# Masking one head of the next unit ahead of VectorE's copies in the third and fifth step of a pair

## The chip, the cores and the metric

The kernel runs on 1 core of one Trainium2 chip. The metric is the device time of one execution in microseconds (us).

## What is computed

Attention over 4 x 8 heads (sequence 576, head dimension 64) with a threshold, then two mixing blocks. Only the attention matters here:

```python
scores = scale * np.matmul(q, k.transpose(0, 1, 3, 2))
thresh = np.max(scores, axis=-1, keepdims=True) - tau
scores = np.where(scores >= thresh, scores, -1000000000.0)
scores = scores - np.max(scores, axis=-1, keepdims=True)
attn = np.exp(scores)
attn = attn / (np.sum(attn, axis=-1, keepdims=True) + 1e-09)
return np.matmul(attn, v).astype(np.float32)
```

Its result goes through a token and a channel mixing block with ReLU, and through a gated convolution block (`x @ w_in`, three taps, sigmoid, `@ w_out`), all in float32.

## The kernel before, in words

Each engine has a program of its own, written out by hand; semaphores are the only link between them. The 32 heads are worked on as 16 **pairs** (k = 0 to 15, `PAIRS` = 16). A pair has 576 rows of queries, cut into five **units** t = 0 to 4: four full ones of 128 rows with two heads each, and a tail (t = 4) in which the 64 last rows of both heads share the 128 partitions, so that it counts as one head. A pair is one call of `body`, with five steps s = 0 to 4. `at.unit(n)` names the unit n steps into the pair; n = 5 and up are those of the next pair. Pairs 0 to 3 and 14 on are written out, 4 to 13 run in a loop, two at a time (an even and an odd one).

The stages of a unit, engine by engine:

- TensorE, `scores` (L1034, tail L1039): the scores of a unit into two pairs of banks of the tensor `score`, one pair per head. Each matmul waits on `max_done`, that is until VectorE has copied the same head of the unit before out of that bank.
- VectorE, `copy_out` (L876): one instruction per head takes the scores out of PSUM, scales and negates them into `negs`, and leaves the row's extreme in `neg_max`. It waits on `s_done` (the scores are there) and on `mask_done` (the buffer of two units ago is free).
- ScalarE, `exp_unit` (L624, L627): one exponential per head as soon as its copy is done, and behind the last the threshold `thresh` of the unit (one instruction for both heads), which signals `thr_done`.
- VectorE, `mask` (L893): one instruction per head compares `negs` with `thresh`, multiplies with the exponential, writes `prob` and adds up the row. It waits on `thr_done`, on `exp_done` for its head, and on `tail_turned` or `t_done`, by which TensorE says that it has turned the `prob` of two units ago.
- TensorE, `turn_probs` (L1060, tail L1069 to L1077): transposes `prob` head by head, each head when its mask is done (`mask_done`), into `turn_x` and `turn_y`. `turn_tails` (L1114) turns the columns of the tail.
- ScalarE, `drain_turned_probs` (L641): copies them to `probT`. Then TensorE multiplies with V in the next pair (`times_v`, L1129), and the result is turned, normalised (VectorE `normalise` L916, ScalarE `normalise_short` L695) and turned back.

In step s of a pair TensorE makes the scores of unit s + 2 and then turns unit s; VectorE copies unit s + 2 out and then masks unit s + 1; ScalarE drains unit s and then does the exponentials of unit s + 2. Behind this, the token mixing of two pairs is spread over the pairs: from k = 3 on in the odd ones its first product (`mix_hidden`, L1181), from k = 4 on in the even ones the second (`mix_out`, L1210). GpSimd splits the weights and the attention's results into high and low parts meanwhile (L440, L454, L477, L491, L498) and adds (L506).

VectorE's body sets the order of the work around the change:

```python
if two:
    copy_out(two)
if s == 4 and at.units:
    invert_sums(at)
if one:
    mask(one)
```

Of the kernel before, what the change touches and what calls it, by code (L numbers as in the profile page):

```python
# [25 lines left out]
def build(nc, qk_in, v_in, tau, w_tok1, w_tok2, w_ch1, w_ch2, w_in, conv_w, w_out, out):  # L26
# [11 lines left out]
    FULL = S // P  # L38
    TAIL = S - FULL * P
    NT = FULL + 1  # L40
# [154 lines left out]
    with ctx:  # L195
# [12 lines left out]
        def sem(name):  # L208
            return ctx.enter_context(nc.semaphore(name))
# [17 lines left out]
        thr_done = sem("thr_done")  # L227
        exp_done = sem("exp_done")
        mask_done = sem("mask_done")
        t_done = sem("t_done")  # L230
        tail_turned = sem("tail_turned")
# [6 lines left out]
        sum_done = sem("sum_done")  # L238
# [75 lines left out]
        def tiles_to(g, t):  # L314

            return TILES * g + min(2 * t, TILES)

        def slot_of(k, t):

            return (NT * k + t) % 2  # L320
# [536 lines left out]
        def _(dve):  # L857
# [9 lines left out]
            def copy_out(unit):  # L867

                g, k, t = unit
                i = slot_of(k, t)  # L870
                if NT * k + t >= 2:
                    before = (g, t - 1) if t >= 1 else (g - 1, FULL)
                    dve.wait_ge(mask_done, tiles_to(*before))
                dve.wait_ge(s_done, NT * g + t + 1)
                for h in range(2 if t < FULL else 1):
                    nc.vector.tensor_scalar(negs[:, i, h, :].rearrange("p (c s) -> p c s", c=2), raw_of[h], neg_scale[:, 0:1], None, ALU.mult, ALU.min,  # L876
                                            accum_out=neg_max[:, i, h:h + 1]).then_inc(max_done, 1)

            def mask(unit):

                g, k, t = unit
                i = slot_of(k, t)
                if NT * k + t >= 2:
                    if t == 1:
                        dve.wait_ge(t_done, NT * g)
                    else:
                        dve.wait_ge(tail_turned, FULL * g + max(t - 1, 0))
                if t == 0 and k >= 1:
                    dve.wait_ge(sum_done, g)
                dve.wait_ge(thr_done, NT * g + t + 1)  # L890
                for h in range(2 if t < FULL else 1):
                    dve.wait_ge(exp_done, tiles_to(g, t) + h + 1)
                    nc.vector.scalar_tensor_tensor(out=prob[:, i, h * S:(h + 1) * S], in0=negs[:, i, h, :],  # L893
                                                   scalar=thresh[:, i, h:h + 1], in1=exps[i][:, h, :],
                                                   op0=ALU.is_le, op1=ALU.mult,
                                                   accum_out=rowsum[:, 2 * t + h:2 * t + h + 1]).then_inc(mask_done, 1)

            def add_to_sums(at):

                dve.wait_ge(mask_done, TILES * (at.g + 1))  # L900
                nc.vector.tensor_scalar(rowsum_pos[:, :], rowsum[:, :], 1e-9, None, ALU.add).then_inc(sum_done, 1)

            def invert_sums(at):

                dve.wait_ge(sum_done, at.g + 1)
                nc.vector.reciprocal(rinv[at.par][:, :], rowsum_pos[:, :]).then_inc(inv_done, 1)

            def normalise(pair, k):

                dve.wait_ge(xa_done, pair + 1)  # L910
                dve.wait_ge(inv_done, pair + 1)
                if k >= 1:
                    dve.wait_ge(x_split, pair)
                    dve.wait_ge(xt_done, pair)
                halves = 2 * FULL
                nc.vector.tensor_tensor(x32[:, 0:FULL, :].rearrange("p t (h c) -> p (t h) c", h=2),  # L916
                                        out_t[:, :].rearrange("p (n c) -> p n c", c=D),
                                        rinv[k % 2][:, 0:halves].unsqueeze(2).broadcast_to([P, halves, D]), ALU.mult) \
                    .then_inc(x_done, 1)

            def split_first_u():
                dve.wait_ge(pv_done, PAIRS)
                for i in range(2):
                    k = slice(i * KM // 2, (i + 1) * KM // 2)
                    dve.wait_ge(u_hi_first, i + 1)
                    nc.vector.tensor_tensor(ul[0][:, k, :], uy[:, 0, k, 0:CHUNK], uh[0][:, k, :].bitcast(F32), ALU.subtract) \
                        .then_inc(u_lo_first, 1)

            first, second = (0, 0, 0), (0, 0, 1)
            copy_out(first)  # L930
            copy_out(second)
            mask(first)

            def body(at):
                for s in range(NT):
                    two, one = at.unit(s + 2), at.unit(s + 1)
                    if two:
                        copy_out(two)
                    if s == 4 and at.units:
                        invert_sums(at)  # L940
                    if one:
                        mask(one)
                    if s == 1 and at.k == PAIRS:
                        split_first_u()
                    if s == 3 and at.pv:
                        normalise(at.g - 1, at.k - 1)
                    if s == 3 and at.units:
                        add_to_sums(at)

            bodies(dve, body)  # L950


# [455 lines left out]
```

## Time and profile before

| | |
|---|---|
| median of 3 runs | 846.94 us (846.65 to 847.15) |
| the profiled execution | 847.35 us |
| its span, first to last instruction | 845.5 us |
| mean granted TensorE clock | 0.996 |
| TensorE matmuls busy | 823.7 us, 97% |
| VectorE busy | 417.7 us, 49% |
| ScalarE busy | 413.3 us, 49% |
| GpSimd busy | 257.5 us, 30% |
| L893, the masks | 144 times, 129.1 us, mean 929 ns |
| L876, the copies | 144 times, 112.7 us, mean 816 ns |
| L624, the exponentials | 144 times, 104.7 us |

Times in the profile count from the span's start. The pairs take the first 330 us or so, the channel mixing and the convolution block the rest. The granted clock is given as a share of 2.4 GHz: 1.00 is 2.4 GHz, 0.50 is 1.2 GHz. In a timeline a row is an instruction (or a run of equal ones, x2, x8): its start, its duration, and in brackets how long the engine was idle before it and what ended that. Durations include the time in the pipeline, so the next instruction of an engine can start a little before the end of the one before.

### The profile page before, as it was taken

Reading aid. Unit: us, or ns where it says so; the run is one execution under the profiler, and the core shown is the slowest. Engines: PE = TensorE matmul, PEld = TensorE weight load, DVE = VectorE, ACT = ScalarE, POOL = GpSimd, SP = SyncE. Lnnn points to the kernel's source line nnn. Section 1 sums busy time; section 2 is a strip of 40 time slices with the busy share of each in tenths; the row PEclk is TensorE's granted clock in tenths of the full one; section 3 lists DMA queues with packets and bytes.
Section 4 is the critical chain, followed back from the end, with each engine's and each line's share of the span. In section 5 each row is a group of like instructions: output and inputs, shape, how many; then the busy total and the mean of one; then the engine's idle time right before and its main releaser. Section 6 shows DMA issues by size and latency. Waiting matters only on the chain.

```text
span 845.5 us, 15190 instructions
## 1 busy us (share of the span) xinstructions
PE 823.7 (97%) x5656; PEld 670.9 (79%) x5656; DVE 417.7 (49%) x829; ACT 413.3 (49%) x914; POOL 257.5 (30%) x202
## 2 busy tenths in 40 slices
PE   8989999999999998899999999999999999999998
PEld 4657777777777767788888888888899999898996
DVE  6887878878878774401211211211214819155380
ACT  5877888878878884211211211211114727265461
POOL 0251223223323224460200200110391726428170
PEclk9999999999999999999999999999999999999999
DMA  9311111111111204000000000000320010100101
GB/s 267 110 47 48 49 48 47 47 47 47 47 47 49 61 2 150 1 1 0 1 1 1 0 1 1 1 0 1 137 63 2 1 51 1 50 13 0 50 0 62
DMA packets 20906, 32.70 MB, mean 39 GB/s; under 512 B 4416, under 2 KB 11136, under 8 KB 20864
## 3 DMA queue, kind: packets, MB, share of 16 engines
q1 hardware_dynamic: 20864, 32.13, 11.8%
q8 instruction: 28, 0.46, 0.2%
q14 instruction: 14, 0.11, 0.0%
HBM read 27.41 MB, written 4.72 MB: 38 GB/s over the span
## 4 chain that ended last, share of the span: by engine, by line
PE 92%; DVE 3%; ACT 2%; issue 2%; DMA 1%; POOL 0%; ACTq 0%; SPq 0%; DVEq 0%; POOLq 0%
PE score L1238 17%; PE score L1353 12%; PE score L1034 7%; PE out_t L1253 4%; PE turn_y L1253 4%; PE mixed L1253 4%; PE turn_x L1253 4%; PE out_t L1129 4%; PE out_t L1338 4%; PE mixed L1129 4%; PE mixed L1181 3%; PE turn_x L1060 3%; PE turn_y L1338 3%; PE mixed L1338 3%; PE turn_x L1338 3%
## 5 line engine op out<-in xcount | busy, mean ns | idle before, releaser
L956 DVE SCALAR_TENSOR_TENSOR h<-score,h 128x512 fp32r<-128x512 f32 (+1 forms) x60 | 38.3, 638 | 243.5 <-ACT h L726 243.5
L726 ACT ACTIVATE h<-score 128x512 fp32r<-128x512 f32 (+1 forms) x60 | 33.3, 555 | 250.5 <-PE score L1238 250.5
L876 DVE TENSOR_SCALAR_CACHE_REDUCE negs<-score,neg_scale 128x576 f32<-128x576 f32 x144 | 112.7, 816 | 60.1 <-PE score L1034 44.8
L893 DVE SCALAR_TENSOR_TENSOR prob<-negs,thresh,exps 128x576 f32<-128x576 f32 x144 | 129.1, 929 | 0.3 <-ACT thresh L627 0.3
L624 ACT ACTIVATE exps<-negs,neg_max 128x576 f32<-128x576 f32 x144 | 104.7, 772 | 1.9 <-DVE negs L876 1.2
L1034 PE MATMUL score<-qk 64*128 64x288 f32 x512 | 85.6, 435 | 2.6 <-DVE negs L876 2.1
L1238 PE MATMUL score<-uh,w1l 128*128 128x512 f32 (+1 forms) x240 | 86.8, 368 | 0.0
L1238 PE MATMUL score<-uh,w1h 128*128 128x512 f32 (+1 forms) x240 | 86.8, 368 | 0.0
L1238 PE MATMUL score<-ul,w1h 128*128 128x512 f32 (+1 forms) x240 | 86.8, 368 | 0.0
L592 POOL TENSOR_TENSOR zl<-z,zh 128x512 fp32r<-128x512 f32 x32 | 54.2, 1693 | 98.7 <-ACT zh_t L814 98.7
L1034 PEld LDWEIGHTS score<-qk 64*128 64x128 f32 x512 | 47.4, 189 | 28.8 <-issue 13.7
L514 POOL TENSOR_TENSOR ul<-uy,uh 128x256 fp32r<-128x256 f32 (+6 forms) x7 | 16.7, 2398 | 161.7 <-ACT uh L713 161.7
L996 DVE SCALAR_TENSOR_TENSOR conv<-hpad,cw,conv 128x576 f32<-128x576 f32 x32 | 27.2, 849 | 77.4 <-ACT conv L827 77.3
L1060 PEld LDWEIGHTS turn_x<-ident,prob 64*128 64x128 f32 x512 | 41.1, 139 | 20.1 <-issue 14.6
L641 ACT ACTIVATE probT<-turn_x 128x512 f32<-128x512 f32 x64 | 38.1, 596 | 35.4 <-PE turn_y L1060 34.4
L1353 PE MATMUL score<-yl,wih 128*128 128x288 f32 x256 | 54.8, 296 | 0.0
L1353 PE MATMUL score<-yh,wih 128*128 128x288 f32 x256 | 54.8, 296 | 0.0
L1353 PE MATMUL score<-yh,wil 128*128 128x288 f32 x256 | 54.8, 296 | 0.0
L1238 PEld LDWEIGHTS score<-uh,w1l 128*128 128x128 f32 x240 | 45.3, 189 | 7.6
L1238 PEld LDWEIGHTS score<-uh,w1h 128*128 128x128 f32 x240 | 45.2, 189 | 7.5
L1238 PEld LDWEIGHTS score<-ul,w1h 128*128 128x128 f32 x240 | 45.2, 188 | 7.4
L1060 PE MATMUL turn_x<-ident,prob 64*128 64x64 f32 x512 | 45.9, 225 | 5.1 <-DVE prob L893 3.0
(184 smaller groups left out, 1968.7 us busy)
## 6 DMA issues: line engine op xcount, KB each, us to landing
qk<-in_qk SPq DMA_DIRECT2D x16, 640.0 KB, 3.9
vm<-in_v SPq DMA_DIRECT2D x16, 320.0 KB, 4.2
result<-ostage SPq DMA_DIRECT2D x16, 256.0 KB, 2.1
w1f<-in_moe_w_ch SPq DMA_DIRECT2D x4, 768.0 KB, 10.8
w2f<-in_moe_w_ch SPq DMA_DIRECT2D x4, 768.0 KB, 7.5
wif<-in_moe_w_in SPq DMA_DIRECT2D x1, 2048.0 KB, 7.9
wof<-in_moe_w_out SPq DMA_DIRECT2D x8, 256.0 KB, 2.6
wt2f<-in_moe_w_tok SPq DMA_DIRECT2D x1, 576.0 KB, 9.4
```

Source lines behind the costliest of these rows:

```text
L592: nc.gpsimd.tensor_tensor(zl[:, t, :], z32[:, t % 2, 0:MAIN], zh[:, t, :].bitcast(F32), ALU.subtract)
L624: nc.scalar.activation(exps[i][:, h, :], negs[:, i, h, :], ACT.Exp, bias=neg_max[:, i, h:h + 1], scale=-1.0).then_inc(exp_done, 1)
L876: nc.vector.tensor_scalar(negs[:, i, h, :].rearrange("p (c s) -> p c s", c=2), raw_of[h], neg_scale[:, 0:1], None, ALU.mult, ALU.min, accu ...
L893: nc.vector.scalar_tensor_tensor(out=prob[:, i, h * S:(h + 1) * S], in0=negs[:, i, h, :], scalar=thresh[:, i, h:h + 1], in1=exps[i][:, h, ...
L956: nc.vector.scalar_tensor_tensor(out=h3[:, n % RING, 1, 0:w], in0=hidden_banks[n % 4][:, 0:w], scalar=0.0, in1=h3[:, n % RING, 0, 0:w].bit ...
L1034: mm = nc.tensor.matmul(score[:, 2 * h + c, 0:HALF], qT[par][rows, t * P:(t + 1) * P], kT[par][rows, halves[c]])
L1060: mm = nc.tensor.transpose(turn[r][:, to:to + D], prob[rows, i, k_at:k_at + P], ident[rows, rows])
L1129: nc.tensor.matmul(bank[mine, 0:HALF], vm[par][:, kt, mine], probT[par][:, h, kt, c * HALF:(c + 1) * HALF], start=(kt == 0), stop=False, s ...
L1238: mm = nc.tensor.matmul(hidden_banks[n % 4][:, 0:w], wt[:, c, kt, :], x[:, kt, 0:w], start=(i == 0), stop=(i == 3 * KM - 1))
L1253: mm = nc.tensor.matmul(sum_banks[mt][:, 0:w], wt[:, c, o:o + P], h3[:, n % RING, part, 0:w], start=(c == 0 and i == 0), stop=(c == KC - 1 ...
L1338: mm = nc.tensor.matmul(bank, z, wt[:, kt, :], start=(kt == 0 and n == 0), stop=(kt == KF - 1 and n == 2))
L1353: mm = nc.tensor.matmul(in_banks[c % 2][:, i, 0:HALF], wt[:, kt, c * P:(c + 1) * P], y[:, kt, i * HALF:(i + 1) * HALF], start=(n == 0), st ...
```

## The change

`mask` gets an argument `heads`. The waits that belong to the unit as a whole are made only in the call that has head 0. In steps s = 2 and s = 4, where there is a next unit, VectorE now calls `mask(one, (0,))` ahead of `copy_out(two)` and `mask(one, (1,))` at the old place. In step 2 that unit is t = 3, and the copy between is that of the tail, one instruction. In step 4 it is unit 0 of the next pair, and between come the two copies of that pair's unit 1 and the small `invert_sums`. The other steps, and the other engines' programs, are as before.

```diff
-            def mask(unit):
+            def mask(unit, heads=(0, 1)):
 
                 g, k, t = unit
                 i = slot_of(k, t)
-                if NT * k + t >= 2:
-                    if t == 1:
-                        dve.wait_ge(t_done, NT * g)
-                    else:
-                        dve.wait_ge(tail_turned, FULL * g + max(t - 1, 0))
-                if t == 0 and k >= 1:
-                    dve.wait_ge(sum_done, g)
-                dve.wait_ge(thr_done, NT * g + t + 1)
-                for h in range(2 if t < FULL else 1):
+                if 0 in heads:
+                    if NT * k + t >= 2:
+                        if t == 1:
+                            dve.wait_ge(t_done, NT * g)
+                        else:
+                            dve.wait_ge(tail_turned, FULL * g + max(t - 1, 0))
+                    if t == 0 and k >= 1:
+                        dve.wait_ge(sum_done, g)
+                    dve.wait_ge(thr_done, NT * g + t + 1)
+                for h in heads if t < FULL else (0,):
                     dve.wait_ge(exp_done, tiles_to(g, t) + h + 1)
...
                 for s in range(NT):
                     two, one = at.unit(s + 2), at.unit(s + 1)
+                    ahead = one and s in (2, 4)
+                    if ahead:
+                        mask(one, (0,))
                     if two:
                         copy_out(two)
                     if s == 4 and at.units:
                         invert_sums(at)
                     if one:
-                        mask(one)
+                        mask(one, (1,) if ahead else (0, 1))
```

How VectorE's instructions then stand. First place: pair 0, from step 2 to step 4, before. `exps1_79` belongs to units of odd number, `exps0_71` to even ones (in pair 0); L876 are the copies and L893 the masks, `rowsum_pos` and `rinv` the sums and their inverses.

```order
L876 TENSOR_SCALAR negs_70,neg_max_55<-score,neg_scale_54 128x576
L893 SCALAR_TENSOR_TENSOR prob_75,rowsum_58<-negs_70,thresh_56,exps1_79 128x576 x2
L876 TENSOR_SCALAR negs_70,neg_max_55<-score,neg_scale_54 128x576 x2
L893 SCALAR_TENSOR_TENSOR prob_75,rowsum_58<-negs_70,thresh_56,exps0_71 128x576
L901 TENSOR_SCALAR rowsum_pos_59<-rowsum_58 128x9
L876 TENSOR_SCALAR negs_70,neg_max_55<-score,neg_scale_54 128x576 x2
L906 RECIPROCAL rinv0_60<-rowsum_pos_59 128x9
L893 SCALAR_TENSOR_TENSOR prob_75,rowsum_58<-negs_70,thresh_56,exps1_79 128x576 x2
```

The same place in the changed kernel, where the masks are at L894:

```order
L894 SCALAR_TENSOR_TENSOR prob_75,rowsum_58<-negs_70,thresh_56,exps1_79 128x576
L876 TENSOR_SCALAR negs_70,neg_max_55<-score,neg_scale_54 128x576
L894 SCALAR_TENSOR_TENSOR prob_75,rowsum_58<-negs_70,thresh_56,exps1_79 128x576
L876 TENSOR_SCALAR negs_70,neg_max_55<-score,neg_scale_54 128x576 x2
L894 SCALAR_TENSOR_TENSOR prob_75,rowsum_58<-negs_70,thresh_56,exps0_71 128x576
L902 TENSOR_SCALAR rowsum_pos_59<-rowsum_58 128x9
L894 SCALAR_TENSOR_TENSOR prob_75,rowsum_58<-negs_70,thresh_56,exps1_79 128x576
L876 TENSOR_SCALAR negs_70,neg_max_55<-score,neg_scale_54 128x576 x2
L907 RECIPROCAL rinv0_60<-rowsum_pos_59 128x9
L894 SCALAR_TENSOR_TENSOR prob_75,rowsum_58<-negs_70,thresh_56,exps1_79 128x576
```

One mask of unit 3 now stands ahead of the tail's copy, and one of the next pair's unit 0 ahead of two copies. Second place: the same in pair 2, with the normalising instruction (`x32`) in between, in the changed kernel.

```order
L894 SCALAR_TENSOR_TENSOR prob_75,rowsum_58<-negs_70,thresh_56,exps1_79 128x576
L876 TENSOR_SCALAR negs_70,neg_max_55<-score,neg_scale_54 128x576
L894 SCALAR_TENSOR_TENSOR prob_75,rowsum_58<-negs_70,thresh_56,exps1_79 128x576
L876 TENSOR_SCALAR negs_70,neg_max_55<-score,neg_scale_54 128x576 x2
L894 SCALAR_TENSOR_TENSOR prob_75,rowsum_58<-negs_70,thresh_56,exps0_71 128x576
L917 TENSOR_TENSOR x32_81<-out_t,rinv1_61 128x512
L902 TENSOR_SCALAR rowsum_pos_59<-rowsum_58 128x9
L894 SCALAR_TENSOR_TENSOR prob_75,rowsum_58<-negs_70,thresh_56,exps1_79 128x576
L876 TENSOR_SCALAR negs_70,neg_max_55<-score,neg_scale_54 128x576 x2
```

The moved mask of step 4 stands directly behind the sums of the pair that ends, and ahead of both copies.

## Rows read from the trace of the kernel before

**Rows 1.** chain that ended last, 18 to 30 us, by line (cut where it is printed)
```profile
by line: DVE prob L893 35.5%; DVE negs L876 23.3%; PE score L1034 16.2%; issue 13.3%; PE out_t L1129 5.3%; PE mixed L1129 4.0%; PE turn_x L1060 2.8%; DVE rinv L906 1.1%; PE turn_y L1060 1.0%; DVEq L892 0.4%; PE turn_x L1069 0.3%; PE mixed L
```

**Rows 2.** waits, 70 to 318 us: engine, line, waited for, total us, times, longest
```profile
DVE negs L876 <- PE score L1034: 39.4, 43, 1.8
```

**Rows 3.** TensorE by stretches: core 0: us, PE busy (x), PEclk, DMA share, GB/s
```profile
58.10:60.10 2.00, 0.48 (x9) 1.00 0.79 315
60.10:66.80 6.70, 6.39 (x38) 0.50 0.01 2
70.00:318.00 248.00, 243.55 (x2358) 1.00 0.14 46
...
349.50:351.10 1.60, 0.00 (x1) 1.00 0.00 0
```

**Rows 4.** timeline, VectorE, pair 0: start us, us, engine, line, operation, tiles, [idle before]
```profile
19.94 0.82 DVE L876 TENSOR_SCALAR_CACHE_REDUCE negs<-score,neg_scale 128x576 f32<-128x576 f32 x1
22.29 0.82 DVE L876 TENSOR_SCALAR_CACHE_REDUCE negs<-score,neg_scale 128x576 f32<-128x576 f32 x1
25.27 0.82 DVE L876 TENSOR_SCALAR_CACHE_REDUCE negs<-score,neg_scale 128x576 f32<-128x576 f32 x1 [0.47 <-PE score L1034]
```

**Rows 5.** timeline, ScalarE, pair 0
```profile
19.78 0.29 ACT L627 ACTIVATE thresh<-neg_max,tau_pos 128x2 f32<-128x2 f32 x1
22.89 0.60 ACT L641 ACTIVATE probT<-turn_x 128x512 f32<-128x512 f32 x1 [0.24 <-PE turn_y L1060]
23.86 1.44 ACT L624 ACTIVATE exps<-negs,neg_max 128x576 f32<-128x576 f32 x2
25.19 0.29 ACT L627 ACTIVATE thresh<-neg_max,tau_pos 128x2 f32<-128x2 f32 x1
```

**Rows 6.** timeline, TensorE, pair 0 and the start of pair 1
```profile
20.91 1.24 PE L1034 MATMUL score<-qk 64*128 64x288 f32 x8
26.15 1.97 PE L1034 MATMUL score<-qk 64*128 64x288 f32 x8 [0.71 <-DVE negs L876]
28.98 0.71 PE L1129 MATMUL out_t<-probT,vm 128*64 128x288 f32 x4
```

**Rows 7.** timeline, VectorE and ScalarE, end of pair 1
```profile
37.27 0.82 DVE L876 TENSOR_SCALAR_CACHE_REDUCE negs<-score,neg_scale 128x576 f32<-128x576 f32 x1 [1.78 <-PE score L1039]
43.41 0.80 DVE L876 TENSOR_SCALAR_CACHE_REDUCE negs<-score,neg_scale 128x576 f32<-128x576 f32 x1
...
43.12 0.28 ACT L627 ACTIVATE thresh<-neg_max,tau_pos 128x2 f32<-128x2 f32 x1
```

**Rows 8.** timeline, pair 2, steps 2 and 3: VectorE, GpSimd, TensorE
```profile
55.90 0.82 DVE L876 TENSOR_SCALAR_CACHE_REDUCE negs<-score,neg_scale 128x576 f32<-128x576 f32 x1 [1.38 <-PE score L1039]
56.65 1.87 DVE L893 SCALAR_TENSOR_TENSOR prob<-negs,thresh,exps 128x576 f32<-128x576 f32 x1
...
53.99 1.78 POOL L454 TENSOR_TENSOR wt2l<-wt2f,wt2h 128x576 fp32r<-128x576 f32 x1
56.49 1.41 POOL L454 TENSOR_TENSOR wt2l<-wt2f,wt2h 128x576 fp32r<-128x576 f32 x1
...
60.41 0.34 PE L1060 MATMUL turn_x<-ident,prob 64*128 64x64 f32 x1 [1.32 <-DVE prob L893]
66.19 1.68 PE L1034 MATMUL score<-qk 64*128 64x288 f32 x8
```

**Rows 9.** timeline, steady pairs: VectorE, ScalarE, TensorE
```profile
181.81 0.82 DVE L876 TENSOR_SCALAR_CACHE_REDUCE negs<-score,neg_scale 128x576 f32<-128x576 f32 x1 [0.43 <-PE score L1034]
194.77 0.82 DVE L876 TENSOR_SCALAR_CACHE_REDUCE negs<-score,neg_scale 128x576 f32<-128x576 f32 x1 [0.40 <-PE score L1039]
...
181.44 0.28 ACT L627 ACTIVATE thresh<-neg_max,tau_pos 128x2 f32<-128x2 f32 x1
...
184.47 1.24 PE L1034 MATMUL score<-qk 64*128 64x288 f32 x8
...
197.91 0.33 PE L1114 MATMUL mixed<-ident,prob 128*128 128x128 f32 x1 [0.23 <-ACT x L695]
```


## The prediction, made before the changed kernel ran

> **What bounds the kernel now.** I read four views, in this order.
>
> First, the chain that ended last, by stretch. From 18 to 30 us (pair 0 into pair 1) its time lies on VectorE: masks 35.5%, copies 23.3%, against 16.2% for the score matmuls [rows 1]. That holds for the first three pairs; from pair 3 on the next view speaks.
>
> Second, the waits. From 70 to 318 us VectorE stands idle before 43 of its copies, 39.4 us in all, until TensorE has made the scores [rows 2]. There TensorE is the bound, busy 243.55 of 248 us at clock 1.00 [rows 3]. Behind 318 us nothing is masked any more, and nothing in the order changes.
>
> Third, TensorE's clock. It is 1.00 (2.4 GHz) in all other stretches shown, but 0.50 (1.2 GHz) from 60.1 to 66.8 us, in pair 2. Just before it fell, from 58.1 to 60.1 us, TensorE was busy 0.48 of 2.00 us [rows 3]: it waited for masks, 1.32 us before the transposes at 60.41 [rows 8].
>
> Fourth, the timelines around the two steps that change. In them a copy's start is followed by the next VectorE start 0.75 us later (55.90 to 56.65) [rows 8]; I take 0.75 us for an undisturbed copy or mask.
>
> **What the change does.** No instruction is added or removed. In step s = 2 the mask of unit 3, head 0, goes in front of the tail unit's single copy; in step s = 4 the mask of the next pair's unit 0, head 0, goes in front of the two copies of its unit 1. The waits move with the first mask: for the exponentials, for the threshold (L627, which ScalarE makes only after both heads' exponentials) and for the turned tails. Whatever that mask waits for, the copies behind it now wait for too, and TensorE waits for the copies (it may overwrite a score bank only then), as does ScalarE. No DMA and no queue of SP or GpSimd is reordered.
>
> **Pair 0, step 2.** The threshold of unit 3 ends at 19.78 + 0.29 = 20.07 [rows 5]. The mask starts at 20.1, the copy at 20.85 instead of 19.94 [rows 4]: +0.9. The scores behind a copy start 0.88 us after its start (25.27 to 26.15) [rows 4, 6], so those of 20.91 move to 21.75 and end 1.24 later at 23.0 [rows 6]; the copies of 22.29 [rows 4] start at 23.0, +0.7. Unit 3's transposes no longer wait for its second head and end 0.6 later than before. ScalarE follows them.
>
> **Pair 0, step 4.** From ScalarE's first copy at 22.89 to the end of the threshold at 25.19 + 0.29 = 25.48 is 2.6 us [rows 5]. Moved by 0.6 the threshold ends at 26.05; mask at 26.1, copies at 26.85 instead of 25.27: +1.55. The scores of 26.15 start at 27.7 and end at 27.7 + 1.97 = 29.65 [rows 6]. Of this 0.6 comes back: the second head's mask, formerly last, is now over before the scores are, so the transposes run without a break and the product with V, at 28.98 before [rows 6], starts at 29.95. TensorE is the bound behind it. **Pair 0: +0.97.** Bounds: +0.6 if ScalarE is not held back, +1.55 if nothing comes back.
>
> **Pair 1.** In step 2 the mask fits into the 1.78 us idle before 37.27: no copy is later. In step 4 the threshold ends at 43.12 + 0.28 = 43.40, the mask takes until 44.15, and the copies of 43.41 come 0.75 later [rows 7]. Against that stands the second mask, which comes about 0.75 earlier behind them, and the transposes that waited for it. I take **-0.1**, bounds -0.3 and +0.75.
>
> **Pair 2.** The idle time before 55.90 is 1.38 us, but GpSimd is at work from 53.99 to 55.77 [rows 8]. The mask at 56.65 took 1.87 us with a GpSimd instruction under way until 57.90, and ended at 58.52, 0.62 after it [rows 8]: it was held. So the moved mask, free to go in that idle time but behind GpSimd, ends at 55.77 + 0.62 = 56.4, and the copy comes at 56.4 instead of 55.90. The Trainium skill ("SBUF — State Buffer", "SBUF: two separate sides") says that VectorE with two SBUF inputs and GpSimd take a shared port pair exclusively, the loser blocked for the whole instruction; the rows agree (the mask ends after GpSimd, not slowed in proportion). This rule speaks against the change here: without it the mask would be free at 55.6, and the copy not late at all.
>
> The scores behind that copy end at 56.4 + 0.88 + 1.24 = 58.5. The second head's mask ends at 58.0, or, if GpSimd's second instruction gets in first, at 59.3. The transposes that started at 60.41 [rows 8] start at 58.7 to 59.4, and end (another 0.45) at 59.1 to 59.9. From there 2.6 us of ScalarE as in pair 0 [rows 5], 0.75 for the mask and 0.88 to the scores give 63.4 to 64.2, against 66.19 [rows 8] in the half-rate stretch. These scores took 1.68 us; at full rate, but waiting for the second copy as in pair 0, 1.97 [rows 6], so 0.3 is lost again. **Pair 2: -2.5 to -1.7, taken -2.1**, if the clock stays at 1.00.
>
> **Steady pairs.** Step 4: the threshold ends at 181.72, the mask at 182.5, so the copies of 181.81 come 0.7 late. The scores that need them, at 182.5 + 0.88 = 183.4, start only at 184.47 [rows 9]: hidden behind TensorE's own work. Step 2, odd pairs: 0.40 us idle before 194.77 takes 0.75 of mask, the copy is 0.35 late; TensorE then waits 0.23 us for ScalarE before 197.91 anyway [rows 9], which leaves 0.12 at most, for six pairs 0.7. I take **0**, because the second mask, earlier now, gives TensorE slack at the same place; upper end +0.7.
>
> **Sum without the clock:** 0.97 - 0.1 - 2.1 + 0 = -1.2 us.
>
> **The clock.** The new order makes waits of the kind that stood before the fall. In pair 0 TensorE is done with unit 4 some 0.7 us before the scores of 26.15 [rows 6], in the new order (0.6 later) at about 26.1, and gets the next scores at 27.7, of which the second head's start only at 28.45: 2.3 us with some 0.3 busy, emptier than 58.1 to 60.1. In pairs 1 and 2 the same comes again, each wait longer by the 0.75 us of the mask. A stretch like the one before costs half of 6.70 us where TensorE is the bound: 3.3 us [rows 3]. Against it: TensorE was idle 1.60 us from 349.5 to 351.1, and the clock stayed at 1.00 [rows 3]. What no row shows is whether a wait in pair 0 is enough: 0 and 3 x 3.3 are the ends. I take one such stretch, since each of three places is about as likely to bring one as not, and two close together are less so. The Trainium skill ("TensorE: Matmul & The Clock Gate", Part 1) says that activity releases the throttle and idling brings it back. By that page alone the new waits count against the change; the traces give the price.
>
> **Forecast:** -1.2 + 3.3 = +2.1 us. The profiled execution was 847.35 us (span 845.5), 0.4 above the median of 846.94; the difference is put on the median: **849.0 us**.
>
> **Rivals.**
> 1. *No half-rate stretch is left.* Pair 2's wait goes, and the waits of pairs 0 and 1 do not bring the clock down. For it: the 1.60 us idle at 349.5. Against it: the new waits are in two parts with little between. -1.2, so 845.7 us; it decides if the granted clock stays at 1.00 between 26 and 70 us. Not slower.
> 2. *Two or three.* Pairs 0 and 1 both bring it. -1.2 + 6.6 = +5.4, so 852.3 us.
> 3. *The port decides pair 2.* GpSimd gets in before both masks, the transposes still wait past 60 us, and the half-rate stretch stays where it was. Then pair 2 gives only some 0.5 us: 0.97 - 0.1 - 0.5 = +0.4, so 847.3 us.
> 4. *The steady pairs pay.* The 0.7 above, plus as much in the even ones, on top of the forecast: 850.4 us.
>
> **Chances.** Forecast 0.38, rival 1 0.22, rival 2 0.23, rival 3 0.10, rival 4 0.07. A measurement tells about 0.2% (1.7 us) from no change. Faster by more than that needs rival 1 with the better end of each term (0.97 - 0.3 - 2.5 = -1.8), or a smaller loss in pair 0: 0.13. Within 0.2%: the rest of rival 1, rival 3, and that part of the forecast where the half-rate stretch falls partly on waits: 0.36. Slower: 0.51. The range reaches from 845.1 (rival 1, best terms) to 852.7 (rival 2 with a few tenths in the steady pairs).
>
> **What would show it.** In the profile after: the copies of pair 0's step 4 about 1.5 us later; a wait of 1.5 us for a copy before TensorE's scores at 27.7; no wait for a mask near 60 us; one stretch at clock 0.50 between 26 and 75 us; the steady pairs as long as now. I am wrong if the clock never falls, if it falls twice, or if the period of the steady pairs moves.

## The result, and the profile after

The changed kernel takes 850.34 us (median of 6 executions, 849.21 to 852.23) against 846.94 (6 executions, 846.57 to 847.15): ratio 1.0039, 95% interval 1.0028 to 1.0051. It is 3.4 us slower, 0.39%, more than the 0.2% that can be told from no change, and inside the range. The profiled execution took 849.62 us with a span of 847.8, that is 2.3 us more than before in the span.

From the page of the profile of the changed kernel: span, engines, and TensorE's granted clock by fortieths of the span, in tenths.

```profile
span 847.8 us, 15190 instructions
...
PE 822.4 (97%) x5656; PEld 670.0 (79%) x5656; DVE 416.0 (49%) x829; ACT 413.6 (49%) x914; POOL 259.3 (31%) x202
...
PEclk9899999999999999999999999999999999999999
```

The chain that ended last shows where VectorE's order now leaves the time. By line, 18 to 32 us (before, 18 to 30 us: [rows 1], masks and copies first):

```profile
by line: PE score L1038 26.7%; ACT exps L624 19.0%; issue 14.3%; ACT probT L641 11.9%; DVE negs L876 10.7%; PE turn_y L1064 7.1%; PE turn_x L1064 5.1%; DVE prob L894 2.5%; ACT thresh L627 1.5%; PE out_t L1103 0.8%; PE mixed L1103 0.5%; DVEq
```

ScalarE's exponentials (L624) and drains (L641) are now on the path, 19.0% and 11.9%, and the masks only with 2.5%: the moved mask waits for ScalarE, and everything behind it with it.

TensorE by stretches (us, busy, clock, DMA share, GB/s), beside [rows 3]:

```profile
26.40:27.60 1.20, 0.02 (x1) 1.00 0.00 0
27.60:34.30 6.70, 6.22 (x36) 0.50 0.00 1
34.30:70.00 35.70, 31.29 (x300) 1.00 0.17 57
70.00:318.00 248.00, 242.80 (x2372) 1.00 0.14 46
```

The clock falls to 0.50 (1.2 GHz) again for 6.7 us, but now behind pair 0. TensorE had been idle for the 1.2 us before (0.02 busy) when it fell. The stretch at 60 us is gone; from 70 to 318 us the clock is 1.00 and TensorE as busy as before.

Pair 0 on VectorE, the answer to [rows 4] (start us, us; L876 copy, L894 mask):

```profile
20.19 0.82 DVE L894 SCALAR_TENSOR_TENSOR prob<-negs,thresh,exps 128x576 f32<-128x576 f32 x1 [0.25 <-issue]
20.93 0.81 DVE L876 TENSOR_SCALAR_CACHE_REDUCE negs<-score,neg_scale 128x576 f32<-128x576 f32 x1
23.27 0.82 DVE L876 TENSOR_SCALAR_CACHE_REDUCE negs<-score,neg_scale 128x576 f32<-128x576 f32 x1 [0.78 <-PE score L1038]
...
26.46 0.82 DVE L894 SCALAR_TENSOR_TENSOR prob<-negs,thresh,exps 128x576 f32<-128x576 f32 x1 [0.68 <-ACT thresh L627]
27.20 0.81 DVE L876 TENSOR_SCALAR_CACHE_REDUCE negs<-score,neg_scale 128x576 f32<-128x576 f32 x1
```

On ScalarE, the answer to [rows 5]:

```profile
23.66 0.60 ACT L641 ACTIVATE probT<-turn_x 128x512 f32<-128x512 f32 x1 [0.70 <-PE turn_y L1064]
...
25.97 0.29 ACT L627 ACTIVATE thresh<-neg_max,tau_pos 128x2 f32<-128x2 f32 x1
```

On TensorE, the answer to [rows 6]:

```profile
21.90 1.24 PE L1038 MATMUL score<-qk 64*128 64x288 f32 x8 [1.08 <-DVE negs L876]
...
28.08 2.54 PE L1038 MATMUL score<-qk 64*128 64x288 f32 x7 [1.66 <-DVE negs L876]
...
30.42 0.68 PE L1038 MATMUL score<-qk 64*128 64x288 f32 x1
...
31.99 0.75 PE L1133 MATMUL out_t<-probT,vm 128*64 128x288 f32 x2
```

Read them together. Step 2: the mask at 20.19 stands ahead of the tail's copy, which comes at 20.93 instead of 19.94, and TensorE waits 1.08 us for it before the scores at 21.90 (before: 20.91). Step 4: the threshold of 25.97 ends at 26.26, the mask goes at 26.46 after 0.68 us idle, the copies at 27.20 instead of 25.27. TensorE waits 1.66 us, makes the scores from 28.08 at half rate (seven matmuls in 2.54 us, the eighth over at 31.10: 3.02 us instead of 1.97), and is at the product with V at 31.99 instead of 28.98.

Pair 2, step 2, the answer to [rows 8]. VectorE (the mask now first, then the copy, then the second mask):

```profile
58.91 1.54 DVE L894 SCALAR_TENSOR_TENSOR prob<-negs,thresh,exps 128x576 f32<-128x576 f32 x1 [0.33 <-PE out_t L1118]
60.39 0.81 DVE L876 TENSOR_SCALAR_CACHE_REDUCE negs<-score,neg_scale 128x576 f32<-128x576 f32 x1
61.13 1.97 DVE L894 SCALAR_TENSOR_TENSOR prob<-negs,thresh,exps 128x576 f32<-128x576 f32 x1
```

GpSimd:

```profile
58.06 1.78 POOL L454 TENSOR_TENSOR wt2l<-wt2f,wt2h 128x576 fp32r<-128x576 f32 x1
...
61.07 1.41 POOL L454 TENSOR_TENSOR wt2l<-wt2f,wt2h 128x576 fp32r<-128x576 f32 x1
```

TensorE, the second head's transposes, which waited 1.32 us before:

```profile
63.25 0.24 PE L1064 MATMUL turn_x<-ident,prob 64*128 64x64 f32 x1 [0.42 <-DVE prob L894]
```

The moved mask takes 1.54 us and ends at 60.45, 0.61 behind GpSimd's instruction of 58.06 (over at 59.84). The second mask takes 1.97 us, again until 0.62 behind the end of GpSimd's (61.07 + 1.41 = 62.48). The wait of 1.32 us has become 0.42.

The steady pairs, VectorE's waits for scores from 72 to 320 us (before, from 70 to 318 us: [rows 2]):

```profile
DVE negs L876 <- PE score L1038: 40.7, 38, 1.6
```

Nothing has moved there, as the lengths show. I cut every trace at the same four places: the tail's scores of pair 0 (17.74 us before), and the first product with V that belongs to pairs 0, 1, 2 and 15 (before 28.98, 47.61, 68.44 and 322.90 us). In us:

```
                              pair 0   pair 1   pair 2   pairs 3 to 15
before                         11.24    18.63    20.83    254.46
changed                        14.21    19.69    19.09    254.42
difference                     +2.97    +1.06    -1.74     -0.04
```

### The profile page after: what moved, and what is told of

The parts are those of the page before. It is cut to its first block, busy times and chain, and to the rows that moved or that the text cites. A ratio compares the mean times of both kernels' runs of the same rounds, so it can differ in the third digit from the quotient of the medians.

```text
span 847.8 us, 15190 instructions
## 1 busy us (share of the span) xinstructions
PE 822.4 (97%) x5656; PEld 670.0 (79%) x5656; DVE 416.0 (49%) x829; ACT 413.6 (49%) x914; POOL 259.3 (31%) x202
## 4 chain that ended last, share of the span: by engine, by line
PE 93%; ACT 3%; issue 2%; DVE 1%; POOL 0%; ACTq 0%; DVEq 0%; POOLq 0%
PE score L1242 17%; PE score L1357 12%; PE score L1038 8%; PE out_t L1257 4%; PE out_t L1133 4%; PE turn_y L1257 4%; PE turn_x L1257 4%; PE mixed L1257 4%; PE out_t L1342 4%; PE mixed L1133 4%; PE mixed L1185 3%; PE turn_x L1064 3%; PE turn_y L1342 3%; PE mixed L1342 3%; PE turn_x L1342 3%
## 5 line engine op out<-in xcount | busy, mean ns | idle before, releaser
L876 DVE TENSOR_SCALAR_CACHE_REDUCE negs<-score,neg_scale 128x576 f32<-128x576 f32 x144 | 112.5, 815 | 50.7 <-PE score L1038 49.3
L894 DVE SCALAR_TENSOR_TENSOR prob<-negs,thresh,exps 128x576 f32<-128x576 f32 x144 | 128.6, 912 | 13.7 <-ACT thresh L627 10.7
L624 ACT ACTIVATE exps<-negs,neg_max 128x576 f32<-128x576 f32 x144 | 104.8, 772 | 3.2 <-DVE negs L876 2.5
L641 ACT ACTIVATE probT<-turn_x 128x512 f32<-128x512 f32 x64 | 38.2, 596 | 37.9 <-PE turn_y L1064 37.1
L1010 DVE TENSOR_TENSOR z<-hpad,conv 128x576 f32<-128x576 f32 x32 | 49.5, 1548 | 1.1 <-POOL zl_t L594 1.1
```

What stands on the lines that cost most here:

```text
L624: nc.scalar.activation(exps[i][:, h, :], negs[:, i, h, :], ACT.Exp, bias=neg_max[:, i, h:h + 1], scale=-1.0).then_inc(exp_done, 1)
L1010: nc.vector.tensor_tensor(z32[:, t % 2, :], hpad[:, t % 3, 1:S + 1], conv[:, t % 3, :], ALU.mult) \
```

## The experiments

All are timed in rounds with the kernel before on the same chip. "Clock" is the mean granted clock of a whole execution, which every run lists; it counts the stretches only roughly. Profiles with one stretch of 3 to 5 us have 0.997 or 0.998 (e4, e6, e7, e9), with one of 6.7 us 0.996 (before) or 0.995 (changed), with two or three 0.995 to 0.993 (e1, e2, e8, e10), with none 0.999 or 1.000 (e3, e5, e11). I take 0.994 and less for more than one; 0.995 can be either. Every profile ends with 2 to 4 us at half rate, which are left out here. The kernel before spreads too: of 24 executions beside e5 to e8, one at 1.000 took 845.49 us, eighteen at 0.997 to 0.998 took 846.58 to 847.26, five at 0.993 to 0.996 took 848.39 to 848.75. Lengths of the profiled executions, cut as above (e10 is the changed kernel again):

```
      pair 0   pair 1   pair 2   pairs 3-15   half rate in the profile, us
e1     12.95    18.28    18.25    255.99      21.6 to 25, 315 to 320
e2     12.02    20.18    23.28    254.68      47 to 53, 70 to 74
e3     12.75    18.50    19.09    254.39      none
e4     11.24    18.64    18.37    255.65      65 to 69
e5     12.86    18.59    19.18    254.35      none
e6     11.25    18.26    18.25    255.86      314 to 318
e7     11.25    18.26    17.80    255.77      312 to 318
e8     13.22    19.69    18.86    255.87      27 to 31, 48 to 51, 317 to 321
e9     11.24    18.44    19.58    254.42      46 to 51
e10    12.77    19.86    20.78    256.21      47 to 51, 67 to 74
e11    11.24    18.28    17.78    254.38      none
```

**e1, step 2 alone.**

```diff
-                    ahead = one and s in (2, 4)
+                    ahead = one and s == 2
```

> Only step 2 masks ahead; step 4 has its old order. My theory (the loss is the wait that step 4 brings in pair 0 and the half-rate stretch behind it): pair 0 loses about 0.75 us (copies of the next pair 0.7 us later), no wait of 1.6 us before scores, clock at 1.00 throughout the first 70 us, pair 1 gains about 0.5, pair 2 gains 2.0 to 2.8; in all 844.3 to 845.5 us. Rival (the held tail copy of step 2 is what costs, in every odd pair): at least as slow as the changed kernel, 850 us.

Measured: 846.76 us (12 executions, 844.73 to 847.48), ratio 0.9987 (0.9978 to 0.9996). The two executions at clock 1.000 and 0.999 took 844.73 and 844.77, as expected; the median is a miss, since half-rate stretches came where I had expected none. TensorE in step 2 of pair 0, where it waits 1.08 us before the scores of 21.71, by stretches:

```profile
19.00:21.60 2.60, 1.20 (x17) 1.00 1.21 290
21.60:25.20 3.60, 3.49 (x26) 0.56 1.09 317
25.20:80.00 54.80, 50.91 (x485) 1.00 0.17 58
```

The order theory holds for pairs 1 and 2 (-0.35 and -2.58); pair 0's own loss can't be read here, since its +1.71 has the half rate in it. The rival (step 2 costs in every odd pair) falls: 846.76 is far from 850. Pairs 3 to 15 are 1.5 us longer in this profile, with the second half-rate stretch among them; e9 has them without one. The clock part was a miss: the clock fell right behind the 1.08 us wait of step 2, which the changed kernel has too; in the changed kernel's profile it did not fall there.

**e2, step 4 alone.**

```diff
-                    ahead = one and s in (2, 4)
+                    ahead = one and s == 4
```

> Only step 4 masks ahead; step 2 has its old order. My theory: the wait for the threshold stays (pair 0 about +0.45 us by order) and so does the half-rate stretch behind pair 0 (+3.2 us), and pair 2 keeps its wait for the masks near 60 us and does not gain: 850.0 to 851.5 us, and some us more in executions that have a second half-rate stretch. Rival (step 2 costs): 846 to 847 us.

Measured: 852.91 us (6 executions, 851.11 to 854.68), ratio 1.0065 (1.0049 to 1.0081). Slower than the kernel before, as my theory has it and the rival not, but above my 850.0 to 851.5 (its interval meets that of e10, the changed kernel again, so which of the two is slower is not shown): three executions lie at 851.1 to 852.0 (clock 0.993) and three at 853.8 to 854.7 (0.991 to 0.990). TensorE by stretches:

```profile
44.00:46.90 2.90, 1.45 (x6) 0.90 0.00 0
46.90:53.20 6.30, 6.30 (x40) 0.51 0.01 3
...
70.50:73.60 3.10, 3.10 (x28) 0.50 0.00 0
```

Half rate comes at the end of pair 1 and of pair 2, not behind pair 0 where I had put it. By order pair 0 loses 0.78 (0.45 expected). Pair 2 keeps its wait for the mask, 1.33 us before 64.11.

**e3, the waits filled.** The changed kernel, with work nobody reads where TensorE waits.

```diff
+                    if s == 4 and k in (0, 1, 2):
+                        pe.wait_ge(tails_drained, TAILS * (g + 1))
+                        for _ in range(3):
+                            nc.tensor.matmul(mixed[:, 0:HALF], uy_pair[:, 2, 0:P], uy_pair[:, 3, 0:HALF])
...
-            nc.vector.memset(uy_pair[:, 0:2, :], 0.0).then_inc(zeros_set, 1)
+            nc.vector.memset(uy_pair[:, 0:4, :], 0.0).then_inc(zeros_set, 1)
```

> The changed kernel with three matmuls of 288 columns that nobody reads, put where TensorE waits in step 4 of pairs 0, 1 and 2, and nothing else moved. My theory (the clock falls because TensorE idles there): clock 1.00 throughout, 3.2 us faster than the changed kernel's faster executions, 846 to 847 us, and no spread of 2 us between executions. Rival (the clock has nothing to do with these waits, the 3 us are lost in the order itself): 850 us, half-rate stretch still there or loss still there at clock 1.00.

Measured: 848.45 us (11 executions, 847.62 to 848.72), ratio 1.0011 (1.0002 to 1.0020), slower than my 846 to 847. The tail's scores of pair 0 come at 19.16, 1.38 us later than in the changed kernel, behind the longer memset (1.98 instead of 1.02 us); in the other profiles they lie between 17.19 and 18.04. TensorE by stretches:

```profile
0.00:84.00 84.00, 76.39 (x636) 1.00 0.39 119
84.00:318.00 234.00, 228.77 (x2234) 1.00 0.14 44
```

The clock stays at 1.00, and pairs 0 and 1 together take 31.25 us, against 33.90 in the changed kernel with its half-rate stretch: the clock costs **2.65 us** there (2.45 against e5), and the order costs 12.75 - 11.24 = **1.51 us** in pair 0. The rival (850 us, or the 3 us lost without half rate too) did not come true.

**e5, the same without the longer memset**: ten matmuls of 128 columns on the identity.

```diff
+                        for _ in range(10):
+                            nc.tensor.matmul(mixed[:, 0:P], ident[:, :], ident[:, :])
```

> As e3, but the idle time is filled with ten short matmuls on the identity, which needs no zeroed buffers: e3's first copies came 1.4 us late for that reason. My theory: clock 1.00 in the first 80 us, the product with V of pair 1 at 30.5 us (before 28.98, changed 31.99), 2.65 us faster than the changed kernel's faster executions: 846.5 to 847.2 us, 848 us median at most. Rival (half-rate stretch not due to these waits): 849.4 us or more.

Measured: 847.68 us (11 executions, 846.83 to 848.48), ratio 1.0007 (0.9998 to 1.0016). The best, at clock 1.000, took 846.83, where I had put the changed kernel without half rate; six from 0.999 up stay below 847.7, five at 0.997 lie at 847.8 to 848.5, so one stretch still comes in some (where, no profile shows). The median is above my 846.5 to 847.2 and below the 848 that I gave as its limit. Ten matmuls were a little too many, and the scores come a little late behind them (pair 0 12.86). Filling the waits takes 2.7 us off the changed kernel's median, and nothing else was changed. None of the changed kernel's eleven executions has a mean clock above 0.995; of e5's eleven none is below 0.997, of e3's none below 0.998. That the clock falls because TensorE idles in step 4 is shown.

**e4, GpSimd out of the way.** The kernel before.

```diff
                 if k == 2:
+                    scores_start(at, 4)
                     for kt in range(KT):
                         split_weight(wt2h[:, kt, :], wt2l[:, kt, :], wt2f[:, kt, :], wt_split)
```

(the block stands behind `rest_of_w1` instead of ahead of it).

> The kernel before, with GpSimd's split of the second token weight moved in pair 2 from ahead of its w1 part to behind it (step 4), so that it is not at work during the masks of unit 3. My theory (those masks are held by GpSimd, and TensorE's wait for them brings the half-rate stretch at 60 us): the masks take 0.81 us, no wait of 1.32 us, clock 1.00 throughout, 1.5 to 2.5 us faster: 844.4 to 845.4 us. Rival (the masks are late for another reason): 846.9 us and the same stretch.

Measured: 845.91 us (11 executions, 844.28 to 846.46), ratio 0.9977 (0.9968 to 0.9986). VectorE's two masks of pair 2, step 2, and one of step 4, where GpSimd's work now is:

```profile
56.85 0.81 DVE L894 SCALAR_TENSOR_TENSOR prob<-negs,thresh,exps 128x576 f32<-128x576 f32 x1
57.59 0.81 DVE L894 SCALAR_TENSOR_TENSOR prob<-negs,thresh,exps 128x576 f32<-128x576 f32 x1
...
63.04 1.13 DVE L894 SCALAR_TENSOR_TENSOR prob<-negs,thresh,exps 128x576 f32<-128x576 f32 x1
```

They took 1.87 and 1.81 us before. The mask of step 4 is held instead (1.13 us), and in the profile the clock falls there:

```profile
56.00:65.00 9.00, 8.43 (x86) 1.00 0.33 111
65.40:69.00 3.60, 3.54 (x22) 0.53 0.00 0
```

The four executions at 0.999 or 1.000 took 844.28 to 844.59, at the lower end of the range I gave or 0.1 below it; the seven at 0.997 or 0.998 took 845.79 to 846.46, some 1.7 us more, and with them the median misses the range. That GpSimd's work held the masks of step 2 is shown, and pair 2 is shorter by 2.46 us. GpSimd's split was moved, not made smaller, so this does not say what it costs where it now is.

**e8, the threshold early.** The changed kernel, ScalarE's L627 ahead of the second exponential.

```diff
                 for h in range(heads):
                     act.wait_ge(max_done, tiles_to(g, t) + h + 1)
+                    if h == heads - 1:
+                        nc.scalar.activation(thresh[:, i, 0:heads], neg_max[:, i, 0:heads], ACT.Identity,
+                                             bias=tau_pos[:, 0:1]).then_inc(thr_done, 1)
```

> The changed kernel, with ScalarE making the threshold ahead of the second head's exponential. My theory (in step 4 the moved mask, and so the copies, wait for the threshold: 0.68, 0.28 and 0.56 us of idle in pairs 0, 1 and 2): these waits go, the copies of pair 0's step 4 come at about 26.5 instead of 27.2 us, and TensorE's wait before the scores shrinks from 1.66 to about 1.0 us; by order 0.6 to 1.2 us faster, and the half-rate stretch in pair 0 may go too: 846 to 849 us. Rival (the copies are late for the mask's own 0.74 us alone): 849.4 us and above.

Measured: 849.73 us (8 executions, 847.90 to 850.59), ratio 1.0024 (1.0013 to 1.0035). VectorE in pair 0, step 4 (mask, copy):

```profile
25.29 0.82 DVE L895 SCALAR_TENSOR_TENSOR prob<-negs,thresh,exps 128x576 f32<-128x576 f32 x1
26.10 0.82 DVE L877 TENSOR_SCALAR_CACHE_REDUCE negs<-score,neg_scale 128x576 f32<-128x576 f32 x1
```

and TensorE's scores behind them:

```profile
26.98 2.54 PE L1039 MATMUL score<-qk 64*128 64x288 f32 x7 [1.14 <-DVE negs L877]
```

The 0.68 us idle before the mask is gone, the copies come 0.85 us earlier than in the changed kernel (counted from the tail's scores, 17.53 here and 17.78 there), TensorE's wait is 1.14 instead of 1.66 us. So part of the delay was the threshold. But the median is above my 846 to 849 and where the rival had it: the clock still falls, in this profile in pairs 0, 1 and 15. I was wrong that a wait shorter by a third would do. How much the order alone gained can't be read at half rate. What the mask's own 0.74 us costs stays.

**e6, the gain alone**: masks ahead in step 2 of pairs 1 and 2 and nowhere else.

```diff
-                    ahead = one and s in (2, 4)
+                    ahead = one and s == 2 and at.k in (1, 2)
```

> The kernel before with the mask ahead in step 2 of pairs 1 and 2 only. My theory (all of the gain sits there, none in the steady pairs, and pair 0 only loses): pair 0 as before (28.98), pair 1 shorter by 0.35 us, pair 2 by 2.6, no half-rate stretch in the first 80 us, 844.0 to 844.6 us. Rival (the steady pairs gained too): slower than the executions of e1 at clock 1.00, 844.7 us.

Measured: 845.47 us (10 executions, 844.05 to 845.58), ratio 0.9974 (0.9965 to 0.9983). At clock 1.000 it took 844.05, as expected, and that is faster than e1 without half rate, so the rival falls; but the median is above my 844.0 to 844.6. Seven of ten are at 0.997 or 0.998, and in the profile a stretch at half rate comes at 314 us, behind a wait of 0.90 us in pair 15 that the kernel before has too. I had not reckoned with that one. The same wait of 0.90 us stands in all profiles but e11's, and the clock fell behind it in four of them (e1, e6, e7, e8), not in the other eight.

**e9, the steady pairs alone against e6.**

```diff
-                    ahead = one and s in (2, 4)
+                    ahead = one and (s == 2 and at.k >= 1 or s == 4 and at.k >= 3)
```

> The change in all places but those where I say it costs: step 2 from pair 1 on, step 4 from pair 3 on. My theory (thirteen steady pairs neither gain nor lose; the loss is step 2 of pair 0 and step 4 of pairs 0 to 2): the same as e6, which has only pairs 1 and 2: 844.0 to 845.6 us, pairs 3 to 15 together within 0.3 us of before's. Rival (masks ahead of copies cost or gain a little in each steady pair): 1 us or more away from e6.

Measured: 845.40 us (9 executions, 844.31 to 845.86), ratio 0.9974 (0.9964 to 0.9984), the same as e6. Pairs 3 to 15 take 254.42 us, before 254.46. The thirteen steady pairs neither gain nor lose. In this profile the clock is at half rate from 46.9 us, at the end of pair 1, where the order is that of the kernel before and TensorE's longest wait from 43 us on is 0.51 us (busy 2.95 of the 3.90 us from 43.0 to 46.9). So the change's waits are not the only ones that the clock can fall behind.

**e10, the changed kernel again.**

> The changed kernel once more, timed beside the others on one chip, to see how its time goes with its mean granted clock. My theory (each half-rate stretch costs 2 to 2.7 us): times in groups that go with the mean clock, about 849.4 us at 0.995 and 851 to 852 at 0.994 to 0.992; none below 848 us unless the clock is 0.999 or more. Rival (spread has another source): no such order.

Measured: 851.66 us (5 executions, 851.22 to 852.62), ratio 1.0053 (1.0039 to 1.0067). Times go with the clock: 851.22 and 851.43 at 0.994, 851.66 and 851.75 at 0.993, 852.62 at 0.991. None came at 0.995, which three of the first six had (849.21 to 849.62). TensorE by stretches in its profile:

```profile
26.00:30.00 4.00, 2.50 (x28) 1.00 0.01 2
...
47.00:54.00 7.00, 7.00 (x66) 0.76 0.01 2
...
68.00:74.00 6.00, 6.00 (x38) 0.50 0.00 0
```

The same program, and now pair 0 goes by at clock 1.00 (12.77 us: the order alone), with stretches at half rate at the end of pairs 1 and 2. So which of the waits brings it differs from execution to execution. Pair 0's scores of step 4 and the product with V, at full rate:

```profile
27.50 1.73 PE L1038 MATMUL score<-qk 64*128 64x288 f32 x7 [1.66 <-DVE negs L876]
...
29.96 0.71 PE L1133 MATMUL out_t<-probT,vm 128*64 128x288 f32 x4
```

With the tail's scores at 17.19 here and 17.74 before, these scores are 1.90 us late and the product with V 1.53.

**e7 and e11, the best of both.** e6, with GpSimd's first half of the weight behind the masks of unit 2 (`pool.wait_ge(mask_done, tiles_to(g, 3))`) and the second in step 4, and three short matmuls in the waits of step 4 of pairs 0 to 2; e11 also

```diff
+                    if s == 2 and k == PAIRS - 1:
+                        pe.wait_ge(max_done, tiles_to(g, 4))
+                        for _ in range(6):
+                            nc.tensor.matmul(banks[3][:, 0:P], ident[:, :], ident[:, :])
```

> e6 plus GpSimd's two halves of the second token weight placed between the masks of pair 2 (the first behind the masks of unit 2, the second in step 4), plus three short matmuls in the waits of step 4 of pairs 0 to 2. My theory: masks of step 2 in pair 2 not held (0.81 us), clock 1.00, 843.5 to 844.4 us without spread. Rival (pair 2 is already bound elsewhere): as e6.

> e7 with six more short matmuls in TensorE's 0.90 us wait of pair 15, where e7's profile shows a half-rate stretch (clock 0.56 from 312 to 315 us). My theory: this stretch goes too, 843.4 to 844.2 us in nearly all executions, clock 0.999 or 1.000. Rival (that stretch is not due to that wait): as e7, 843.7 to 845.0 us.

Measured: e7 844.24 us (5 executions, 843.69 to 845.00), ratio 0.9964 (0.9951 to 0.9977); e11 844.13 us (5, 843.55 to 844.32), ratio 0.9960 (0.9947 to 0.9974), its five at 0.999 or 1.000. Both medians lie in my ranges, but e7 was to be without spread. e7 by stretches, around pair 15's wait (0.90 us, until 311.13):

```profile
309.00:312.00 3.00, 1.90 (x33) 1.00 0.00 0
312.00:318.00 6.00, 5.85 (x47) 0.72 0.55 197
```

e11, whole:

```profile
0.00:84.00 84.00, 77.56 (x678) 1.00 0.39 119
84.00:300.00 216.00, 213.24 (x2065) 1.00 0.15 48
300.00:330.00 30.00, 27.38 (x243) 1.00 0.30 106
330.00:841.00 511.00, 505.43 (x2707) 1.00 0.05 18
```

With the wait of pair 15 filled, the stretch is not in e11's profile. But three of e7's five executions are at 0.999 or 1.000 as well, so with five of each it is not shown that the six matmuls removed it, nor are the medians apart. Both beat the kernel before by 3 us and the changed kernel by 6.

## Why the prediction was right

By its steps:

- **The bound.** As read: VectorE's order matters in pairs 0 to 2 only. Steady pairs: taken 0, measured -0.04 us over thirteen (e9 confirms).
- **Pair 0, step 2.** Mask at 20.1, copy at 20.85, scores 21.75, copies 23.0; measured 20.19, 20.93, 21.90, 23.27.
- **Pair 0, step 4.** Here the sum was mis-sized. The mask at 26.1 and the copies at 26.85 were 26.46 and 27.20 (the threshold was 0.2 later, and 0.2 passed from its end to the mask's start). So the scores came +1.90 late (e10) where the sum had +1.55. Of this I had "0.6 comes back"; 0.4 did: from the scores' start to the product with V it is 2.46 us in e10, against 2.83 before and the 2.25 of the forecast. +0.97 was forecast, +1.51 to +1.53 measured (e3, e10), just inside the upper bound of +1.55. In the old order the wait for the second head's mask, which was to pay for this, was only 0.16 us (before the transposes of 28.52).
- **Pair 1.** -0.1 forecast, -0.13 (e3) to -0.04 (e5) measured.
- **Pair 2.** -2.5 to -1.7, with the lower end if GpSimd's second instruction got in first. It did, and it is -1.74, not the -2.1 taken. The mask was to end 0.62 us behind GpSimd; it did, to 0.01. The Trainium skill ("SBUF — State Buffer", "SBUF: two separate sides") has VectorE with two SBUF inputs and GpSimd take a shared port pair as an exclusive lock, the one that comes second blocked. These masks agree, and so does e4's, 0.62 us behind GpSimd's instruction of 62.15 to 63.55; only that a mask needs 0.74 us by itself, and ends 0.62 after the lock should be free, is not explained by it.
- **The clock.** One stretch was forecast, at 3.3 us; the profiled execution has one, at 2.65 us (33.90 - 31.25). 3.3 took TensorE to be busy throughout, but in the first 0.5 us of the stretch it was still waiting for VectorE (6.22 of 6.70 us busy, so half is 3.1). Where the other 0.45 went is not shown. The waits of step 4 in pairs 1 and 2 are 1.63 and 1.43 us; in pair 1 that is 1.1 more than the 0.49 before, not the 0.75 of the forecast.

Put together for the profiled execution: 1.5 - 0.1 - 1.7 + 0 + 2.65 = +2.35 us, against the span's +2.3; forecast was +2.1. Pair 0 was taken 0.55 too small, pair 2's gain 0.35 too large and the clock 0.65 too large, and these nearly cancel: that the total comes within 0.3 us is in part luck.

For the median this is not the whole story. By their mean clock of 0.994 or less, three of the first six executions and all five of e10 have more than one stretch: rival 2 ("two or three", 852.3 us, 0.23) is the case in eight of eleven, the forecast in three at most, and the median of all eleven is 851.43 us. 850.34 lies between the two groups: that the first six fell half and half was luck for the forecast, and its range, 845.1 to 852.7, is wide enough to hold rivals 1 and 2 as well. In the two profiles the clock fell in step 4 of each of the three pairs at least once, as forecast; that one stretch is likeliest was wrong. Rival 1, no half rate, never occurred in eleven executions; e5 shows what it would have been, 846.83 us, not the 845.7 I gave, by pair 0 and pair 2 again. Rival 3, that the port keeps the wait at 60 us, did not happen (0.42 us), and rival 4 is excluded.

What stays open: what decides in an execution which wait brings the half rate. The order is the same each time, and waits of 1.08 and 1.66 us (pair 0), 1.63 (pair 1) and 1.43 (pair 2) stand in it.

## What to carry to other kernels

An instruction moved ahead brings its waits with it. Ask of each, not only whether the engine is idle there, but whether what it waits for is done by then and who waits for the instructions now behind it: in pairs 1 and 2 the mask of step 2 filled idle time, in step 4 it made VectorE wait for ScalarE and TensorE for VectorE. Where an order only matters in the ramp of a pipeline, change it there alone (e6 is 5 us better than the same idea everywhere). And price a TensorE wait by what it does to the clock as well: here 1 to 2 us of wait cost up to 2.65 us more, and a few matmuls that nobody reads, put into the waits of step 4, took most of that away (e3, e5).

## What the runs showed of the hardware

- The clock falls on waits that I had passed over as small: 1.08 us in the middle of 2.6 us with 1.20 busy (e1), and 0.90 us in pair 15 (e7). Elsewhere it did not fall: TensorE idle for 1.60 us at 349.5 us in the kernel before, 1.66 us in pair 0 of e10, 0.90 us in pair 15 of eight profiles.
- The same program has its half-rate stretches at different places in different executions (the first profile behind pair 0, e10 at the end of pairs 1 and 2), and its time differs by up to 3.0 us with them (849.21 to 852.23 in the first six), while the kernel before repeats within 0.7 us in eighteen of the 24 executions beside e5 to e8.
- A mask held by GpSimd ended 0.62 (before), 0.61 and 0.62 us (changed) behind the end of GpSimd's instruction (58.52, 60.45 and 63.10 us), however long it had taken (1.87, 1.54 and 1.97 us).
